# A convolution and a token mixer on one core: TensorE work done as one matmul over the whole array, or as two over its halves

## What is computed

```python
w = softmax(weight)                       # 8 heads x 7 taps
y[s, h, g] = sum_k w[h, k] * x[s + k - 6, h, g]
W_tok = (y @ w_q) @ (y @ w_k).T / sqrt(64)
out   = relu(W_tok @ y) @ w_out
```

## Time and profile before

| | |
|---|---|
| median of 3 runs | 174.63 us |
| the profiled execution | 174.48 us, span 172.5 us |
| TensorE busy | 157.5 us, 3213 matmuls |
| VectorE, ScalarE busy | 120.9, 121.3 us |
| GpSimd busy | 30.3 us |
| HBM read and written | 27.56 and 25.95 MB |

### The profile page before, as it was taken

How to read it: one execution, slowest core, us unless ns; L and a number is a source line. 1 busy time by engine, 2 the same in 40 slices (tenths; PEclk the granted TensorE clock), 3 DMA queues, 4 the chain that set the end, 5 groups by cost and what they waited for, 6 DMA issues and landing times.

```text
span 172.5 us, 7076 instructions
## 1 busy us (share of the span) xinstructions
PE 157.5 (91%) x3213; PEld 118.5 (69%) x3213; DVE 120.9 (70%) x212; ACT 121.3 (70%) x206; POOL 30.3 (18%) x39
## 2 busy tenths in 40 slices
PE   4869979998999999998997999999999999999960
PEld 1548748876777777786786877887778777784630
DVE  5866757677766868676896536779677688499650
ACT  2254678877879666885966979678779887758840
POOL 7999452522302120000000000000000000000000
PEclk9999999999999999999999999999999999999995
DMA  2999999999999999999999999986365436096896
GB/s 24 148 184 187 207 189 192 193 217 293 261 338 220 326 238 294 278 218 341 278 292 193 285 287 284 267 209 240 155 237 191 184 135 256 13 370 249 305 336 243
DMA packets 48157, 40.36 MB, mean 234 GB/s; under 512 B 37632, under 2 KB 40960, under 8 KB 48128
## 3 DMA queue, kind: packets, MB, share of 16 engines
q0 software_dynamic: 36128, 13.61, 66.4%
q1 hardware_dynamic: 12000, 26.31, 42.0%
HBM read 27.56 MB, written 25.95 MB: 310 GB/s over the span
## 4 chain that ended last, share of the span: by engine, by line
PE 88%; ACT 3%; issue 3%; DVE 2%; DMA 2%
PE ps L891 15%; PE ps L742 15%; PE ps L310 10%; PE ps L909 8%; PE ps L314 7%; PE ps L311 5%; PE ps L673 5%; PE ps L833 5%; PE ps L705 5%; PE ps L845 5%; PE ps L709 4%; PE ps L315 3%; DMA wt_f<-in_weight_dram 2%; PE ps L337 1%; ACT rt L862 1%
## 5 line engine op out<-in xcount | busy, mean ns | idle before, releaser
L614 ACT CAST y<-ps 122x864 bf16<-122x864 f32 (+3 forms) x50 | 38.2, 793 | 8.7 <-PE ps L311 8.3
L862 ACT ACTIVATE rt<-ps 128x1024 bf16<-128x1024 f32 (+3 forms) x49 | 36.9, 777 | 9.7 <-PE ps L833 7.0
L929 ACT COPY out_sb<-ps 128x768 f32<-128x768 f32 (+1 forms) x41 | 29.9, 740 | 14.3 <-PE ps L909 14.1
L929 DVE COPY out_sb<-ps 128x768 f32<-128x768 f32 (+1 forms) x31 | 27.6, 897 | 14.4 <-PE ps L909 13.4
L507 POOL DMA_DIRECT2D xw<-in_x_dram x34 | 29.9, 894 | 30.8 <-issue 30.0
L742 PE MATMUL ps<-y 122*64 122x64 bf16 (+3 forms) x840 | 33.8, 221 | 0.8 <-DVE mbd L356 0.7
L742 PEld LDWEIGHTS ps<-y 122*64 122x64 bf16 (+1 forms) x840 | 30.4, 110 | 5.5 <-issue 1.4
L311 PE MATMUL ps<-xw,band 128*64 128x432 bf16 (+3 forms) x144 | 30.5, 323 | 1.6 <-issue 1.6
L310 PE MATMUL ps<-xw,band 128*64 128x432 bf16 (+3 forms) x144 | 30.7, 323 | 0.0
L641 DVE COPY ytl<-ps 128x976 bf16<-128x976 bf16 (+1 forms) x40 | 23.2, 590 | 6.2 <-PE ps L315 6.2
L863 DVE TENSOR_SCALAR rt<-ps 128x512 bf16<-128x512 f32 (+3 forms) x31 | 20.8, 674 | 7.6 <-PE ps L833 5.8
(11 more groups left out here) (101 smaller groups left out, 223.3 us busy)
## 6 DMA issues: line engine op xcount, KB each, us to landing
out_dram<-out_sb SPq DMA_DIRECT2D x28, 768.0 KB, 7.1
xw<-in_x_dram POOLq DMA_DIRECT2D x7, 816.0 KB, 41.6
xw<-in_x_dram POOLq DMA_DIRECT2D x7, 768.0 KB, 42.5
out_dram<-out_sb SPq DMA_DIRECT2D x8, 384.0 KB, 4.3
xw<-in_x_dram POOLq DMA_DIRECT2D x2, 432.0 KB, 8.4
out_dram<-out_sb SPq DMA_DIRECT2D x8, 96.0 KB, 5.8
xw<-in_x_dram POOLq DMA_DIRECT2D x1, 384.0 KB, 5.3
xw<-in_x_dram POOLq DMA_DIRECT2D x8, 45.8 KB, 29.0
```

The lines of the kernel that those rows point to most:

```text
L614: return e.copy(dst, src) if op.engine == "ACT" else e.tensor_copy(dst, src)
L862: return e.activation(dst, src(), AF.Relu)
L929: return e.copy(dst, src) if op.engine == "ACT" else e.tensor_copy(dst, src)
```

## The change

An operation that is marked as able to (`whole=True`: conv, tr_lo, turn, m, mix_hi with two token halves, fin_other) may stand in the table with the letter F in place of P. It then runs on TensorE as one matmul over all 128 rows and columns instead of two over column halves. For fin_other F means that its matmul contracts all 128 lower channels at once, one for each of the two token sets; its fin then does the upper channels alone. 84 of the table's 960 entries have an F: 22 tr_lo, 24 fin_other, 17 conv, 11 mix_hi, 6 turn, 4 m. The table is written anew, so that the whole order differs, with banks and the choice between ScalarE and VectorE. The second half of the tokens is transposed from token 2074, a chunk's edge, instead of 2176, and wq reads it 102 columns further on (`AHEAD`). The wide identity, the fp32 transposes of the run-up and the run-up's wait for `own` go.

```diff
-39G 2D 14G 12D 7D 38G 1D 40G 16P 3D 41G 9D 42G 0S 43G 57G 58G 59G 60G 61G 15D 62G 6D 63G 64G 65G 66G 67G 68G
...
+43S 44S 94F6 95D 99A 92F3 93A 118F5 102F0 104P2 106P6 107D 143P 100F3 101D 80G 81G 82G 144P 114F6 108F1
...
+            if engine == "F":
+                assert op.whole
+                op.mode = FULL
...
-    def halves(e, out, lhsT, rhs, **k):
-
+    def halves(e, out, lhsT, rhs, mode=COL2, **k):
+
+        if mode == FULL:
+            return e.matmul(out, lhsT, rhs, **k)
         e.matmul(out[0:64], lhsT[:, 0:64], rhs, **k)
         return e.matmul(out[64:128], lhsT[:, 64:128], rhs, **k)
 
-    def turn_halves(e, out, in_, identity):
+    def turn_halves(e, out, in_, identity, mode=COL2):
+        if mode == FULL:
+            return e.transpose(out, in_, identity)
...
-                if n == 6 and i >= 3:
-                    wide = RUNUP[:, :].bitcast(F32)
-                    last = e.transpose(bank(GB)[0:96, 0:122], wide[0:122, 0:96], WIDE[0:122, 0:122])
...
-    def make_own(e, op):
-        e.tensor_copy(WIDE[:, :], IDENT[:, :])
-        return e.tensor_reduce(OWN[:, :], IDENT[:, :].rearrange("p (k i) -> p i k", i=16), AX.X, ALU.add)
-
-    own = add("DVE", make_own, 400, needs=[ident], vt=-8.92)
-    run_2.needs.append(own)
+    own = add(
+        "DVE",
+        lambda e, op: e.tensor_reduce(OWN[:, :], IDENT[:, :].rearrange("p (k i) -> p i k", i=16), AX.X, ALU.add),
+        200, needs=[ident], vt=-8.92)
...
+    BK = SPLIT // CW
+    AHEAD = SPLIT - BK * CW
+    NP = NCC - BK
     HG = 6
-    hi_cols = [(c * CW, min((c + HG) * CW, SPLIT)) for c in range(0, -(-SPLIT // CW), HG)]
+    hi_cols = [(k * CW, min(k + HG, NP) * CW) for k in range(0, NP, HG)]
...
-                    ps[64 * i : 64 * i + DH, 0:n], WQH[:, i, :], YTH[:, q0 : q0 + n], start=False, stop=True
+                    ps[64 * i : 64 * i + DH, 0:n], WQH[:, i, :], YTH[:, q0 + AHEAD * i : q0 + AHEAD * i + n], start=False, stop=True
...
+            if op.mode == FULL:
+                return e.matmul(
+                    bank(op.bank)[0 : 64 * nh, 0:n],
+                    MBD[:, mb, 0 : 64 * nh],
+                    WQT[:, wqb, q0 : q0 + n],
...
-                for lo in (False, True):
+                for lo in (False, True) if op.then.mode == ROW2 else (False,):
...
-                        p = slice(64 - 64 * a, 128 - 64 * a)
+                        p = slice(64 - 64 * a, 128 - 64 * a) if op.mode == ROW2 else slice(0, 128)
```

More of the change, by code:

```diff
@@ L20 @@
[L20 to L24, removed]
@@ L71, with __init__ @@
     n = 0
-    def __init__(self, engines, emit, ns, needs=(), after=(), banks=0, drains=None, vt=0.0, mode=COL2, tail=0.0):
+    def __init__(self, engines, emit, ns, needs=(), after=(), banks=0, drains=None, vt=0.0, mode=COL2, tail=0.0, whole=False):
         self.engines = (engines,) if isinstance(engines, str) else tuple(engines)
@@ L86, in __init__ @@
         self.mode = mode
+        self.whole = whole
         self.tail = tail
@@ L197 @@
 Op.apart = None
+Op.then = None
 def bass_lightweight_conv__then__hypermixer_token_mlp_kernel(
@@ L331, in emit @@
             last = None
-            for i in range(n):
-                if n == 6 and i >= 3:
-                    wide = RUNUP[:, :].bitcast(F32)
-                    last = e.transpose(bank(GB)[0:96, 0:122], wide[0:122, 0:96], WIDE[0:122, 0:122])
-                else:
-                    last = e.matmul(bank(GB)[:, 0:512], RUNUP[:, 0:128], RUNUP[:, :], start=True, stop=True)
+            for _ in range(n):
+                last = e.matmul(bank(GB)[:, 0:512], RUNUP[:, 0:128], RUNUP[:, :], start=True, stop=True)
             return last
@@ L605, in gen_conv @@
             mm = add(
-                "PE", conv, mm_ns(n * GRP, 2), needs=[*load[b, gi], bands[hp], zero_x, zero_x0], after=[*ev_needs, run_3], banks=nb, vt=vt, kind="conv")
+                "PE", conv, mm_ns(n * GRP, 2), needs=[*load[b, gi], bands[hp], zero_x, zero_x0], after=[*ev_needs, run_3], banks=nb, vt=vt, whole=True, kind="conv")
             def evac(e, op, hp=hp, mm=mm):
@@ L633, in tr_lo @@
                 w, o = width[c], c * CW - t0
-                last = turn_halves(e, ps[:, o : o + w], Y[0:w, yb, c, 0:LO], IDENT[0:w, 0:w])
+                last = turn_halves(e, ps[:, o : o + w], Y[0:w, yb, c, 0:LO], IDENT[0:w, 0:w], op.mode)
             return last
-        mm_l = add("PE", tr_lo, 57 * n, needs=needs, after=free, banks=1, vt=vt, kind="tr_lo")
+        mm_l = add("PE", tr_lo, 57 * n, needs=needs, after=free, banks=1, vt=vt, whole=True, kind="tr_lo")
         evs = [
@@ L654, in gen_transpose_hi @@
         q0, qz = hi_cols[g]
-        ends = (qz, min(qz, S - SPLIT))
-        starts = (0, SPLIT)
-        parts = [chunks_in(starts[i] + q0, starts[i] + ends[i]) for i in range(2)]
-        lead = [starts[i] + q0 - parts[i][0] * CW for i in range(2)]
-        at = max(lead)
-        needs = [*{id(r): r for p in parts for c in p for r in y_done[b, c]}.values(), ident]
+        ks = range(q0 // CW, qz // CW)
+        cs = sorted({k + i * BK for k in ks for i in range(2)})
+        needs = [*{id(r): r for c in cs for r in y_done[b, c]}.values(), ident]
         free = yth_read.get((b - 1, g), [])
@@ L697, in gen_wq @@
         wfree = wq_read.get((b - 2, j), [])
-        gs = [g for g, (a, z) in enumerate(hi_cols) if a < q0 + n and z > q0]
+        gs = [g for g, (a, z) in enumerate(hi_cols) if a < q0 + n + AHEAD * (nh - 1) and z > q0]
         turned = [r for g in gs for r in yth_done[b, g]]
@@ L767, in gen_mix_weights @@
             "PE",
-            lambda e, op: turn_halves(e, bank(op.bank).bitcast(BF16)[:, 0:LO], GSB[:, 64:D], IDENT[:, :]),
-            60, needs=[g_read, ident], banks=1, vt=vt, kind="turn")
+            lambda e, op: turn_halves(e, bank(op.bank).bitcast(BF16)[:, 0:LO], GSB[:, 64:D], IDENT[:, :], op.mode),
+            60, needs=[g_read, ident], banks=1, vt=vt, whole=True, kind="turn")
         turned = add(
@@ L789, in m @@
                     rhs,
+                    mode=op.mode,
                     start=k == 0,
@@ L796, in gen_mix_weights @@
         gsb_read = mm = add(
-            "PE", m, 290, needs=[g_read, turned, *casts_k], after=m_read.get(b - 2, []), banks=1, vt=vt, kind="m")
+            "PE", m, 290, needs=[g_read, turned, *casts_k], after=m_read.get(b - 2, []), banks=1, vt=vt, whole=True, kind="m")
         mb = b % 2
@@ L854, in gen_mix @@
         ml = add("PE", mix_lo, mm_ns(n), needs=[*evm, evq], after=free, banks=nh, vt=vt, mode=ROW2, kind="mix_lo")
-        mh = add("PE", mix_hi, mm_ns(n), needs=[*evm, evq, zero_w], after=free, banks=1, vt=vt, kind="mix_hi")
+        mh = add("PE", mix_hi, mm_ns(n), needs=[*evm, evq, zero_w], after=free, banks=1, vt=vt, whole=nh == 2, kind="mix_hi")
         m_read.setdefault(b, []).extend([ml, mh])
@@ L919, in gen_mix @@
             fl = add(
-                "PE", fin_other, 82.0 * step, needs=[rl, rh, *casts_o], vt=fvt + 0.03, mode=ROW2, kind="fin_other"
+                "PE", fin_other, 82.0 * step, needs=[rl, rh, *casts_o], vt=fvt + 0.03, mode=ROW2, whole=True, kind="fin_other"
             )
+            fh.then = fl
             fl.apart = fh
```

132 lines of the change are left out of this document (67 added, 65 removed).

## The result

The changed kernel takes **170.18 us** (median of four runs, 169.92 to 170.60) against 174.68 for the kernel before on the same chip; the ratio is 0.974, 95% interval 0.971 to 0.977. The time lies outside the range of the forecast, on the other side of no change. The profiled execution's span is 167.7 us instead of 172.5.

What follows compares the result with a forecast made beforehand. TensorE, busy 157.5 of 172.5 us, was taken as the bound. Turns +2.9, high transposes -0.4, output waits -0.7 and lead-in -0.1 summed to +1.7 us: 176.3 us, about 1% slower, range 171.0 to 179.0 us.

Steps and rivals of the forecast that it cites:

- Turns: TensorE's changes of array shape: 26 fewer between halves, 59 new with F, at 0.12 us each; together +2.9 us.
- Rival A: TensorE's turns from halves to whole cost only 0.03 us, so whole groups are a cheap bridge: 171.8 us; chance 30%.
- rival B: Whole transposes on TensorE wait for their weights, 0.08 us each, adding 4.7 us: 181.0 us; chance 8%.
- Columns and high transposes: On TensorE, whole matmuls take the same columns, counted as nothing; 36 high transposes a batch instead of 38 give -0.4 us.
- Waits of the output products: Places where a pair's second output product waits for the first to land fall from 8 to 5: -0.7 us.
- Lead-in: Before the first convolution, no wide identity copy and run-up matmuls without the wait for own-tap sums: -0.1 us.
- The step that failed: Loading whole matmuls' weights 128 columns at once on TensorE was taken as no cost, with up to 4.7 and 1.0 us possible.
- Rival C: The extra turns fall into TensorE's 3.9 us of idle time between 24 and 167 us: 174.5 us, no change; chance 17%.
- The sign of being wrong: The forecast is wrong if TensorE's idle time in the middle changes by more than 2 us either way.

Runs made afterwards that it cites:

- e2: The changed kernel's code with the order, banks and engines of the kernel before and no whole matmul: 172.57 us, ratio 0.990 to the kernel before.
- c1: The changed kernel's order with other operations marked whole, 100 turns instead of 120 and 60 more instructions before the loads end: 172.52 us.
- l1: The kernel before, with x loaded in full only for two of the eight batches: 169.61 us, ratio 0.971.
- e1: The changed kernel with all 84 F in its table turned into P, so the same order with no whole matmul: 179.02 us, ratio 1.025 to the kernel before.
- h1: The order of the kernel before, with the new lead-in and high transposes, and 44 operations marked whole: 170.94 us, ratio 0.980.
- n1: The changed kernel with 550 already met semaphore waits added on TensorE before 112 us, matmuls untouched: 210.4 to 216.4 us in four runs.
- n2: The changed kernel with 550 already met semaphore waits added on TensorE between 118 and 148 us, after the loads of x: 207.2 us.

## Why the prediction was wrong

- *Turns* (+2.9 us): right in price and sign. In the two traces the turns and the slow pair behind them take 9.9 and 13.6 us, +3.8; 0.9 more, since the ten turns in the first batch are counted in it. Rival A (0.03 a turn into whole) is out, and that its 171.8 us lies near the measured time is luck; so is rival B out: whole transposes come every 0.053 us, not 0.08. For these the Trainium skill, "TensorE: Matmul & The Clock Gate", Back-to-back issue gap, has about 81 ns (at 128 columns); this trace, with 53 ns at 122 columns, does not agree, and the measurement decides.
- *Columns and high transposes* (-0.4): -0.3 in the trace.
- *Waits of the output products* (-0.7): waits in the last products fall from 2.6 to 2.0 us, -0.6.
- *Lead-in* (-0.1): too small. The first convolution stands at 7.86 instead of 8.38, -0.5; in e2, with the old order, it was -1.1.
- **The step that failed** is "Their weights are loaded 128 columns at once instead of twice 64 side by side ... I take nothing", together with the reading of the earlier trace rows that TensorE had only 2.8 us to gain between 24 and 158 us. I priced the halved number of instructions by the pace of weight loads alone, as a possible cost, and never as a gain; the instructions have to be fetched, and that was late by 6 us in the kernel before. Outside the last products the waits fall by 5.8 us. With that, the two traces' sum is 3.8 - 0.3 - 0.6 - 0.5 - 5.8, -0.8 of small steps and -0.6 behind the last matmul: -4.8 us, the difference of the spans.
- *Rival C* had waits absorbing turns, at 174.5 us. Waits did fall, but not by hiding turns; and "no change" was not the outcome.
- *The sign of being wrong* that I had set for this, idle time in the middle changed by more than 2 us, would not have shown it: by the busy rows it went from 2.8 to 1.6 us, since busy time hides most of a short stop.

The page had a hint before the run: "issue 3%" in the chain is about 5 us in which an engine waited for nothing shown, and I read past it. The share alone does not tell, for the page of the new kernel still has 2% and no late step at a block's edge; the places do.

Not settled: whether a packet that begins late was asked for late or stood behind the loads (the records show when it begins, not when it was asked for), and what sets the 2.4 us from there to the first instruction. One caveat on the new trace: 8 of the 11 whole high mixings have no record in it, so that single sums of mine are good to some 0.3 us.

## What to carry to other kernels

On an engine that is busy over 90%, count instructions as well as columns: where idle time is put down to "issue" in the middle of one tile's work, see whether such places lie a multiple of 256 instructions apart, and whether bulk loads run beside them. Then compare the work in each block with the time that a block takes to come, here 6.3 us under loads. Then a form with fewer instructions can pay even if it costs the engine time of its own: here 550 fewer before the loads ended were worth more than 3.8 us of turns. And marks or orders around such an edge are not to be judged one by one: c1 saved the turns that it should and lost more, in part because a block's edge had moved to a place with too little work behind it.

## What the runs showed of the hardware

- TensorE's instructions come in packets of 16 KB, 256 instructions. A packet begins 3.6 to 4.5 us after the first instruction of the block ahead of its own while software-issued loads take 66% of the DMA engines' time (before), and 0.2 to 2.1 us after it without them (l1, 25 to 110 us). A late block starts 2.2 to 2.7 us after its packet; the stops were 0.1 to 2.7 us.
- A turn costs 93 to 98 ns beyond the columns between any two of whole, column halves and row halves, whichever way (medians of 12 to 28 turns of each kind in the new kernel), and 13 to 30 ns more in the step behind it.
- A wait of 2.5 us in TensorE's stream was followed by 3.4 us at half clock (e1), and one of 2.0 us too (h1).
- Semaphore waits that are already met stand 0.106 us apart on TensorE (n1, n2).
